# A fused attention and mixture-of-experts kernel: x combinations and low halves on VectorE, zeros on ScalarE, one bias per head pair in the lead, warming transposes between the first scores

## What is computed

```
scores = scale * q @ k.T + slope_h * (-|i - j|), kept where 0 <= i - j < 128
x      = softmax(scores) @ v                      -> 2304 x 512
p      = domain_probs / (sum + 1e-9)
y      = sum over 4 experts e of p[:, e] * (relu(x @ w1[e]) @ w2[e])     (w1: 512 x 1024)
logits = y @ phi (32 slots); dispatch by a softmax over the rows
         to 8 experts of 4 slots each; combine by a softmax over the slots -> 2304 x 512
```

## Time and profile before

| | |
|---|---|
| median of three runs | 997.35 us |
| the profiled execution | 997.73 us, of which its span is 995.9 us |
| TensorE busy (PE) | 957.9 us, 96% |
| GpSimd busy (POOL) | 659.6 us, 66% |
| VectorE busy (DVE) | 596.0 us, 60% |
| ScalarE busy (ACT) | 446.6 us, 45% |
| mean granted TensorE clock | 0.982 of full |

### The profile page before, as it was taken

One profiled execution on the slowest core, in us unless ns is written; L12 is line 12 of the kernel. 1 busy time (PEld: TensorE's weight loads), 2 busy tenths in 40 slices (PEclk: granted clock), 3 DMA queues, 4 the chain that ended last, 5 costly groups with the idle time before them and its releaser, 6 DMA issues.

```text
span 995.9 us, 18516 instructions
## 1 busy us (share of the span) xinstructions
PE 957.9 (96%) x6067; PEld 793.7 (80%) x6067; DVE 596.0 (60%) x1175; ACT 446.6 (45%) x943; POOL 659.6 (66%) x587
## 2 busy tenths in 40 slices
PE   8879999999999989999999999989999999999896
PEld 6558888888888878888888888878888899887532
DVE  5895556565565776556566565665655656556602
ACT  4774444444444544444444444634434344432312
POOL 5988676667669796666667668797866676661000
PEclk8799999999999989999999999999999999999998
DMA  8633314214214213314214212119212122137896
GB/s 251 187 92 114 107 43 128 91 42 130 88 48 126 89 43 112 109 43 127 92 42 130 88 46 82 43 50 333 73 56 84 42 84 69 58 104 283 348 377 238
DMA packets 86403, 116.90 MB, mean 117 GB/s; under 512 B 6208, under 2 KB 56896, under 8 KB 86352
## 3 DMA queue, kind: packets, MB, share of 16 engines
q1 hardware_dynamic: 84736, 109.89, 33.9%
q0 software_dynamic: 1616, 6.36, 1.7%
HBM read 111.51 MB, written 4.72 MB: 117 GB/s over the span
## 4 chain that ended last, share of the span: by engine, by line
PE 82%; POOL 7%; DVE 4%; issue 4%; DMA 1%; ACT 1%; DVEq 0%; SPq 0%; POOLq 0%; ACTq 0%
PE banks L1364 36%; PE banks L1346 32%; PE banks L1304 3%; PE banks L1256 2%; POOL h_lo L665 2%; PE banks L1497 1%; PE banks L1524 1%; PE banks L1278 1%; POOL ws_lo L656 1%; PE banks L1280 1%; DVE w_lo L1043 1%; POOL w_lo L656 1%; PE banks L1237 1%; DMA out<-slot_w 1%; PE banks L1423 1%
## 5 line engine op out<-in xcount | busy, mean ns | idle before, releaser
L1071 DVE SCALAR_TENSOR_TENSOR acc<-banks,prob,acc 128x512 f32<-128x512 f32 x288 | 215.5, 748 | 191.4 <-PE banks L1364 191.2
L1364 PE MATMUL banks<-w_hi,h_hi 128*128 128x512 f32 x576 | 227.1, 394 | 5.0 <-POOL h_lo L665 2.7
L1364 PE MATMUL banks<-w_hi,h_lo 128*128 128x512 f32 x576 | 229.2, 398 | 0.0
L1364 PE MATMUL banks<-w_lo,h_hi 128*128 128x512 f32 x576 | 228.4, 396 | 0.0
L665 POOL TENSOR_TENSOR h_lo<-c,h_hi 128x384 fp32r<-128x384 f32 x144 | 149.8, 1057 | 103.4 <-ACT c L842 103.2
L840 ACT ACTIVATE h_hi<-c 128x384 fp32r<-128x384 f32 x144 | 75.0, 521 | 169.5 <-PE banks L1364 100.6
L656 POOL TENSOR_TENSOR ws_lo<-w_sum,ws_hi 128x1024 fp32r<-128x1024 f32 x48 | 117.0, 2438 | 33.4 <-ACT ws_hi L816 33.4
L1346 PE MATMUL banks<-xT_hi,ws_hi 128*128 128x384 f32 x384 | 131.3, 342 | 3.1 <-POOL ws_lo L656 3.1
L1346 PE MATMUL banks<-xT_lo,ws_hi 128*128 128x384 f32 x384 | 129.1, 336 | 0.0
L1346 PE MATMUL banks<-xT_hi,ws_lo 128*128 128x384 f32 x384 | 128.8, 335 | 0.0
L1364 PEld LDWEIGHTS banks<-w_hi,h_hi 128*128 128x128 f32 x576 | 108.7, 189 | 23.9 <-issue 9.2
(11 more groups left out here) (169 smaller groups left out, 1612.5 us busy)
## 6 DMA issues: line engine op xcount, KB each, us to landing
w_raw<-w SPq DMA_DIRECT2D x96, 512.0 KB, 4.1
slot_w<-m2w SPq DMA_DIRECT2D x4, 2048.0 KB, 11.9
v_b<-v_n SPq DMA_DIRECT2D x24, 256.0 KB, 5.4
slot_early<-m2w POOLq DMA_DIRECT2D x3, 2048.0 KB, 12.5
slot_early<-m2w SPq DMA_DIRECT2D x3, 2048.0 KB, 12.3
v_a<-v_n SPq DMA_DIRECT2D x20, 256.0 KB, 5.3
out<-slot_w SPq DMA_DIRECT2D x9, 512.0 KB, 4.7
q_b<-q_t SPq DMA_DIRECT2D x12, 288.0 KB, 4.6
```

Of the source, the lines that this page charges most:

```text
L1071: dve.scalar_tensor_tensor(acc[:, tile, :], ps_y[tt % 2][:, :], prob[:, tile, bass.ds(e, 1)], acc[:, tile, :], ALU.mult, ALU.add).then_inc ...
L1364: ins = pe.matmul(ps_y[tt % 2][:, :], hh[:, f, tt * P:(tt + 1) * P], wp[u % 2][:, f, :], start=m == 0, stop=m == 3 * FT - 1)
```

## The change

VectorE takes over all x combinations and all seven x low halves, in the lead and in both transitions; one semaphore, s_xlo, counts them. In the lead it combines `kk` = 0 at v = 13 (behind w2_rest), and splits at v = 15 to 21. In the transitions it combines at t = 5 and t = 28, in front of that piece's `add_out` or `add_product`, and splits behind each x_hi. ScalarE writes the zeros, six ACTIVATEs of 128x512 with scale 0 in place of one memset: in the lead behind the first unit's `hid_hi` and before the first expert, in the transitions at six pieces from t = 44. VectorE waits for all six before the next pass. GpSimd makes one bias table per head pair in the lead (6 in place of 10). TensorE's opening 46 transposes become 8, and 42 more stand behind the first six steps' scores.

```diff
+        FILL = {0: 4, 1: 12, 2: 8, 3: 8, 4: 6, 5: 4}
...
+            n = (v + 9) // ATT
+            return n if (v + 9) % ATT == 0 and 0 < n <= KD + 1 else None
+
+        def bias_buf(n, a, lead):
+
+            return n % 2 if lead else a // 3
...
-        ZERO_AT = 45
+        ZERO_AT = [44, 46, 47, 48, 50, 51]
...  (GpSimd)
-            pair_bias(0, 0, 0)
+            pair_bias(0, 0, 0, 0)
             for v in range(FIRST, LEAD):
-                j = bias_at(v)
-                if j is not None:
-                    pair_bias(j[0] // KD, *j)
+                n = bias_at(v)
+                if n is not None and n <= KD:
+                    pair_bias(n // KD, n, n % 2, place(n - 1, 0))
+                elif n is not None:
+                    pair_bias(1, KD, 1, place(KD, 0))
...
-                if v == 13:
-                    pool.wait_ge(s_oc, FROM + 4)
-                    combine_x(0, slice(0, 1), 0)
-                if v in (16, 18, 20):
-                    x_rest(0, 0, v // 2 * 2 - 15, slice(0, 1))
...
-            for n in (1, 3, 5):
-                x_rest(0, 1, n, slice(1, 2))
             w1_rest(0, 0, 1, 0)
             w1_rest(0, 0, 1, 1)
-            zero(0)
...
-                            if last and t == 3:
-                                pool.wait_ge(s_oc, FROM + 2 * (KD * (p + 1) + 3))
-                                combine_x(p + 1, slice(0, 1), 4 * (2 * p + 1))
-                            if last and t == 28:
-                                pool.wait_ge(s_oc, FROM + 2 * (KD * (p + 1) + 4))
-                                combine_x(p + 1, slice(1, 2), 4 * (2 * p + 2))
-                            if last and t - 1 in X_HI_AT:
-                                n = X_HI_AT.index(t - 1)
-                                if n % 2:
-                                    x_rest(p + 1, p + 2, n, BOTH)
-                            if last and t == ZERO_AT:
-                                zero(p + 1)
...  (ScalarE)
+            def zero(p, tt):
+
+                act.wait_ge(s_xlo, NPROD * (p + 2))
+                act.activation(acc[:, p * NTP + tt, :], ident[:, 0:1].broadcast_to([P, D]), ACT.Copy,
+                               scale=0.0).then_inc(s_zero, 1)
...
+                        if last and p + 1 < PASSES and t in ZERO_AT:
+                            zero(p + 1, ZERO_AT.index(t))
                         if up is not None and k == 0:
                             first_product(*up)
...
             for j in range(4):
                 hid_hi(0, 0, 0, j)
+            for tt in range(NTP):
+                zero(0, tt)
...  (VectorE)
+            def combine_x(p, kk):
+
+                for j, (out_, x, y) in enumerate(COMBS):
+                    if j >= 1:
+                        dve.wait_ge(s_comb, 8 * p + 4 * kk + j)
+                    k = slice(kk, kk + 1)
+                    dve.tensor_tensor(x_quarter(p, out_, k), x_quarter(p, x, k), x_quarter(p, y, k),
+                                      ALU.subtract).then_inc(s_comb, 1)
...
                             n = X_HI_AT.index(t - 1)
-                            if n % 2 == 0:
-                                x_rest(p + 1, p + 2, n, BOTH)
+                            x_rest(p + 1, p + 2, n, BOTH)
+                        if last and p + 1 < PASSES and t in (5, 28):
+                            dve.wait_ge(s_oc, FROM + 2 * (KD * (p + 1) + (3 if t == 5 else 4)))
+                            combine_x(p + 1, (5, 28).index(t))
...
-                if v in (15, 17, 19, 21):
+                if v == 13:
+                    dve.wait_ge(s_oc, FROM + 4)
+                    combine_x(0, 0)
+                if 15 <= v < 15 + NPROD:
                     x_rest(0, 0, v - 15, slice(0, 1))
...
-            for n in (0, 2, 4, 6):
+            for n in range(NPROD):
                 x_rest(0, 1, n, slice(1, 2))
...
-                dve.wait_ge(s_zero, p + 1)
+                dve.wait_ge(s_zero, NTP * (p + 1))
...  (TensorE)
-            keep_warm(46, bank[1])
+            keep_warm(8, bank[5])
             pe.wait_ge(s_zrow, 4)
             for v in range(FIRST, LEAD):
                 j = v + LEAD_S
                 if 0 <= j < LEAD:
                     scores(*step(j), True)
+                if j in FILL:
+
+                    keep_warm(FILL[j], bank[5])
```

More of the change, by code:

```diff
@@ L241, in build @@
         s_comb = sem("s_comb")
-        s_combd = sem("s_combd")
         s_xhi = sem("s_xhi")
-        s_xlod = sem("s_xlod")
-        s_xlop = sem("s_xlop")
+        s_xlo = sem("s_xlo")
         s_w1 = [sem("s_w1_0"), sem("s_w1_1")]
@@ L354, in bias_at, with bias_no @@
         def bias_at(v):
[L356 to L362, removed]
+            n = (v + 9) // ATT
+            return n if (v + 9) % ATT == 0 and 0 < n <= KD + 1 else None
+        def bias_buf(n, a, lead):
+            return n % 2 if lead else a // 3
+        def bias_no(n, a, lead):
+            return n + 1 if lead else KD + 2 + 2 * (n - KD - 1) + a // 3
         SCORE_BANKS = ([3], [6, 0])
@@ L615, in _, with pair_bias @@
                                base=0, pattern=[[1, 2 * WIN]], channel_multiplier=-1).then_inc(s_relm, 1)
-            def pair_bias(p, n, late):
+            def pair_bias(p, n, buf, freed):
                 i = head(p, n)
-                pool.wait_ge(s_neg, FROM + place(n, 0) - (0 if late else 3))
+                pool.wait_ge(s_neg, FROM + freed)
                 pool.nop(nofuse=True)
-                pool.tensor_tensor(bias[late][:, :, :],
+                pool.tensor_tensor(bias[buf][:, :, :],
                                    relm[:, :].unsqueeze(1).broadcast_to([P, 2, BAND + WIN]),
@@ L725, in expert @@
                             if t == 4 and (p + 2 < PASSES or not last):
-                                pair_bias(p + 2 if last else p + 1, n, 0)
+                                pair_bias(p + 2 if last else p + 1, n, 0, place(n, 0) - 3)
                             if t == 30 and (p + 2 < PASSES or not last):
-                                pair_bias(p + 2 if last else p + 1, n, 1)
-                            if last and t == 3:
-                                pool.wait_ge(s_oc, FROM + 2 * (KD * (p + 1) + 3))
-                                combine_x(p + 1, slice(0, 1), 4 * (2 * p + 1))
-                            if last and t == 28:
-                                pool.wait_ge(s_oc, FROM + 2 * (KD * (p + 1) + 4))
-                                combine_x(p + 1, slice(1, 2), 4 * (2 * p + 2))
-                            if last and t - 1 in X_HI_AT:
-                                n = X_HI_AT.index(t - 1)
-                                if n % 2:
-                                    x_rest(p + 1, p + 2, n, BOTH)
-                            if last and t == ZERO_AT:
-                                zero(p + 1)
+                                pair_bias(p + 2 if last else p + 1, n, 1, place(n, 0))
                         for s_ in body_steps(p, e, last, [b + 3 for b in BODY_S], t):
@@ L761, in _ @@
                     pool.wait_ge(s_oc, FROM + PASSES * KD * 2)
-                    pool.wait_ge(s_xlod, 4 * (PASSES + 1))
-                    pool.wait_ge(s_xlop, 3 * (PASSES + 1))
+                    pool.wait_ge(s_xlo, NPROD * (PASSES + 1))
                     for n in range(EARLY):
@@ L906, in _ @@
                     x_hi(0, 0, slice(1, 2))
-                    act.wait_ge(s_combd, 3)
+                    act.wait_ge(s_comb, 7)
                     x_hi(0, 1, slice(1, 2))
-            act.wait_ge(s_combd, 4)
+            act.wait_ge(s_comb, 8)
             for n in range(2, NPROD):
@@ L1005, in mask_min @@
                 w = width(p, a)
-                late = a // 3
+                mine = bias[bias_buf(n, a, lead)]
                 c0 = BAND if is_first(p, a) else 0
@@ L1009, in mask_min @@
                 dve.wait_ge(s_exp, FROM + place(n, a) - 1)
-                dve.wait_ge(s_bias, 2 * n + late + 1)
+                dve.wait_ge(s_bias, bias_no(n, a, lead))
                 dve.nop(nofuse=True)
@@ L1015, in mask_min @@
                         in0=ps_s[:, h, 0:w],
-                        in1=bias[late][:, h, c0:c0 + w], scale=-SCALE, scalar=3e38,
+                        in1=mine[:, h, c0:c0 + w], scale=-SCALE, scalar=3e38,
                         op0=ALU.add, op1=ALU.min, accum_out=negmax[:, a, h:h + 1])
@@ L1118, in _ @@
                     dve.wait_ge(s_oc, FROM + 2 * KD)
-                    for j, (out_, x, y) in enumerate(COMBS):
-                        if j >= 1:
-                            dve.wait_ge(s_combd, j)
-                        dve.tensor_tensor(x_quarter(0, out_, slice(1, 2)), x_quarter(0, x, slice(1, 2)),
-                                          x_quarter(0, y, slice(1, 2)), ALU.subtract).then_inc(s_combd, 1)
-            for n in (0, 2, 4, 6):
+                    combine_x(0, 1)
+            for n in range(NPROD):
                 x_rest(0, 1, n, slice(1, 2))
```

9 lines of the change are left out of this document (3 added, 6 removed).

## The result

Four runs of the changed kernel took 1007.14 to 1011.01 us, a median of 1007.63. Against the runs of before on the same chip (997.53) the ratio is 1.0106, 95% interval 1.0079 to 1.0133: 10 us slower, where 990 was forecast, and outside the range of 979 to 999. The profiled execution took 1007.61 us with a span of 1005.4, against 995.9 before. TensorE's busy time stayed (958.5 us), GpSimd's fell from 659.6 to 609.9, VectorE's rose from 596.0 to 613.3.

What follows compares the result with a forecast made beforehand. TensorE, busy 96%, was taken to lose time in the lead and transitions, where GpSimd is fullest and delays VectorE. Terms: -3.2 - 1.0 + 1.5 + 2.0 - 4.0 - 2.5 = -7.2 us, from 997.7 to 990.5, so 990; range 979 to 999.

Steps and rivals of the forecast that it cites:

- Combinations at t = 5: Both transitions: four VectorE combinations in turn with GpSimd, 4.5 us against 3.5 slack; loss 1 us each, 2 in all.
- The bound of 6 us for both transitions together: Upper end of the 0 to 6 us range given for the loss by the combinations at t = 5.
- Rest of the lead: Lead after the start: GpSimd sheds 9.5 us, VectorE stays about as full; gain 1.0 us, bounds +6 to -7.
- First transition, t = 28 on: ws_lo no longer late, TensorE waits for VectorE in pieces; gain 4.0 us of 7.3, 0.6 if the clock falls.
- I don't expect the clock to fall: First transition from t = 28: no waits like the earlier pair of 1.56 + 2.35 us within 4 us.
- Second transition: Same turns of VectorE and GpSimd without attention beside them; gain 2.5 us of 5.2, bounds 5.2 to -0.9.
- the start: Lead's opening: first scores at 4.8 us instead of 9.7, k_b of the next pair landing at 33.4; gain 3.2 us.
- the zeros: Lead: six ACTIVATEs on ScalarE take 3.1 us ahead of copy u, which has 1.6 slack; loss 1.5 us.
- VectorE becomes the bound: Rival, chance 0.12: seven lead operations cost 10.4 us without relief, plus both clock falls; slower, 1005 us.
- The forecast's own test: The forecast is wrong if VectorE's row sums still take 0.49 us in the mean.
- Its other sign: The forecast is wrong if the transitions show the clock at 0.50.

Runs made afterwards that it cites:

- the cut: Changed kernel with each GpSimd low half of w1 and of the w1 sums issued as four operations of 128x256: 993.0 us, ratio 0.9950.
- the start alone: Kernel before with only the start changed, 8 opening transposes in place of 46 and 42 between the first scores: 999.3 us, ratio 1.0005.
- three kernels: Changed kernel (1007.6 us); it with the transitions' combinations back on GpSimd (1000.9); it with their first combination at t = 3 (1003.4).
- the last three versions: Changed kernel with cut, combination at t = 3, lead's zeros on GpSimd, w2_rest earlier: 987.0 us; plus x low halves and w2_rest later: 985.6; x low halves only: 986.0.

## Why the prediction was wrong

**The step that failed first is "Combinations at t = 5"**: 1 us each was forecast, 6.4 and 1.7 were paid. I priced the four at 1.1 us each, by GpSimd's bias and w1 sums beside them, and called the rest VectorE's slack of 3.5. Two of them in the first transition, and one in the second, met w1's low halves, of 2.4 us each, which I had in the earlier trace rows as the very cause of VectorE's long operations. The bound of 6 us for both transitions together was too low also: it left out that a wait of 4.18 us takes the clock with it. Priced by that mechanism the first transition's are 2 x 2.6 + 2 x 0.9 = 7 us against a slack of 3.5. Moving the four two pieces ahead, or cutting what stands beside them, took the cost away.

**"Rest of the lead"** was to gain 1.0 and lost 4.0 (2.7 - 1.7 for the zeros + 3.0 from the start, with the landmark of 91.39). I counted busy time: what VectorE gets and what it gets back. That sum was even too cautious, 24.59 us and not 28.7. But TensorE doesn't wait for VectorE's sum, it waits for pT, and w2's low half and four combinations stood as one block of 4.8 us in front of it. TensorE's lead over the kernel before, 3.4 us at 36.4, was gone at 55 us, by such waits and by 17 us at half clock (39.0 to 45.8, 49.3 to 59.5) in place of 10 (37.9 to 48.1). It came back in part, 1.2 us at 66.7, and the combination beside GpSimd's w_lo took 2.6. The sum left this out too: it had GpSimd with less to do, and not GpSimd's long operation coming earlier, beside VectorE's old work. Kernels with the same lead differ by 2.4 us there, so a term of 1 us was not to be had from one trace.

**"First transition, t = 28 on"** was to gain 4.0 and lost 0.3. Right: ws_lo was not late, and the waits went to VectorE. Wrong: "two more x_lo at 0.9"; one took 2.92, behind w1's low half, and an old one 2.33. And "I don't expect the clock to fall": it fell behind the wait of 2.26 us for pT, to 0.50 from 373.6 to 376.9. With the cut it gained 1.6, with two low halves behind pT 4.8. **"Second transition"**: 1.6 of 2.5, right in sign and mechanism; 4.2 with the cut.

**Right**: the start (3.0 us at the second k_b landing against 3.2; scores at 4.55; k_b gating at 23.43) and that the new start holds the clock, 1.00 between 10 and 20 us, where it was 0.50 from 14 us on the earlier trace rows. No run has the earlier scores without the filling, so the filling's own share is not shown. By TensorE: Matmul & The Clock Gate, Part 4, in the Trainium skill, transposes wouldn't count; what speaks against that is the opening of the kernel before, where nothing but transposes ran from 2.0 us and each took half as long from 7.2 us on. (The clock of 1.00 in the first row is no measurement of full speed: its 24 transposes in 5 us are at half rate, and the trace has no record of the clock before 7 us.) That the gain is kept to the end was wrong, as the start alone shows. **Right**: the zeros, 1.7 against 1.5.

**The rival "VectorE becomes the bound"** gave 1005, with a chance of 0.12. It had the engine right. That its number came near 1007.6 is luck: it was summed from a VectorE without relief in the lead and two clock falls from t = 28 on, where the runs have relief and the largest loss at t = 5. The mechanism was not in it: I argued against it that "less from GpSimd can't leave the waits as they are". The waits between the two engines did shrink, in the lead by 4 us on the row sums alone, and VectorE was less full there than before. It was late all the same, as its order and its neighbours decide, not its load. The forecast's own test said this too: the mean row sum fell from 0.49 to 0.17 us, which was to prove it right. Its other sign, the clock at 0.50 in the transitions, came true.

What stays open: why the same lead ends 2.4 us apart in three kernels. The granted clock between 12 and 91 us goes with it (0.89, 0.87 and 0.83 for ends of +2.7, +4.7 and +5.1), but with one profiled execution each it isn't shown whether the kernels differ or only the executions. For the same reason it is open how much of the last three versions' gain is in the lead.

## What to carry to other kernels

Before an elementwise operation that reads only SBUF moves to VectorE, look at which GpSimd operation will be in flight at its new place: the longest one there is its price, not its own 0.56 us. Look at the old work too: what GpSimd sheds brings its long operations forward, beside other VectorE work. Cutting GpSimd's long operations is cheap when GpSimd isn't full (65 us more of its busy time bought 14.6 us here) and was worth nothing where it is. And price a moved block by what stands behind it in its in-order queue: in the lead the busy time of both engines fell here, and TensorE was later.

## What the hardware showed that was not expected

A VectorE operation on two SBUF inputs beside GpSimd costs GpSimd's whole remainder, in both sizes tried: one of 128x384 ends 0.42 us behind a GpSimd operation of 2.54 and of 2.37 us, and takes 0.98 to 1.09 us beside ones of 128x256. An add on one small SBUF input pays the same as a tile: a row sum of two elements 2.32 us beside the whole and 0.69 beside the cut, at one place of the kernel before, and the prob_sum add of 128x18 1.95 us. A reduction of 128x72 in SBUF doesn't wait (0.21 us at 36.07), a reciprocal of 128x2 doesn't (0.17 us at 35.98, in the same ws_lo), nor does an operation with one input in PSUM (0.54 us at 358.76). So what a VectorE operation pays is told by its kind and its inputs, not by its size. And 65 us more work on GpSimd, 288 instructions, gave a faster kernel.
